# Channel sums of the last stage: two split products over the whole array, or eight unsplit products over two column halves

## The reference

```
def _moe2_ref(x, w_ch1, w_ch2):
    X = np.fft.fft(x, axis=1)
    X = np.fft.fft(X, axis=2)
    u = x + np.real(X)
    mu = np.mean(u, axis=-1, keepdims=True)
    var = np.mean((u - mu) ** 2, axis=-1, keepdims=True)
    un = (u - mu) / np.sqrt(var + 1e-06)
    ch = np.maximum(un @ w_ch1, 0.0) @ w_ch2
    return (u + ch)
```

## Time and profile before

| | |
|---|---|
| median of 3 runs | 1059.18 us (1058.96 to 1059.49) |
| the profiled execution's own time | 1058.91 us |
| its span, first to last instruction | 1057.1 us |
| PE busy | 1032.0 us, 98% of the span, 6896 matmul records |
| PE weight loads busy | 979.6 us, 93% |
| DVE, ACT, POOL busy | 582.2, 502.3 and 413.9 us |
| granted TensorE clock, mean | 0.998 |

### The profile page before, as it was taken

The page is one execution under the profiler, slowest core; times in us unless marked ns, Lnnn a source line. Parts: engine busy times, 40 slices in busy tenths (PEclk is TensorE's granted clock), DMA queues, the critical chain, the costliest instruction groups (busy, mean ns, idle before and its releaser), DMA issues.

```text
span 1057.1 us, 18202 instructions
## 1 busy us (share of the span) xinstructions
PE 1032.0 (98%) x6896; PEld 979.6 (93%) x6896; DVE 582.2 (55%) x1135; ACT 502.3 (48%) x1252; POOL 413.9 (39%) x363
## 2 busy tenths in 40 slices
PE   6899999999999999999999999999999999999998
PEld 5898899999999999999999999888888888888998
DVE  6998995467875477784465687443124114114111
ACT  5989775656875646875656643221111121111110
POOL 5878784343664434573423247331211211111000
PEclk9999999999999999999999999999999999999999
DMA  8636111023302032301123137102001000100000
GB/s 242 198 89 193 44 47 54 6 85 123 104 25 60 1 123 85 104 25 37 36 79 111 45 123 276 41 1 72 1 1 40 33 1 37 35 1 3 34 1 35
DMA packets 41271, 70.08 MB, mean 66 GB/s; under 512 B 6624, under 2 KB 22368, under 8 KB 40672
## 3 DMA queue, kind: packets, MB, share of 16 engines
q1 hardware_dynamic: 40880, 68.59, 20.5%
q10 hardware_dynamic: 304, 0.33, 0.1%
HBM read 56.50 MB, written 12.41 MB: 65 GB/s over the span
## 4 chain that ended last, share of the span: by engine, by line
PE 84%; DVE 6%; POOL 3%; issue 3%; ACT 3%; DMA 0%; DVEq 0%; SPq 0%; ACTq 0%; POOLq 0%
PE PB L840 21%; PE PB L841 21%; PE PB L842 21%; PE PB L905 8%; PE PB L867 6%; PE PB L885 5%; DVE probs L1442 3%; PE PB L907 1%; DVE neg_s L1427 1%; ACT probsT L1169 1%; PE PB L990 1%; ACT exps L1160 0%; POOL k_lo L696 0%; POOL q_hl L689 0%; DMA k_raw<-kT_dram 0%
## 5 line engine op out<-in xcount | busy, mean ns | idle before, releaser
L1386 ACT ACTIVATE h_hi<-PB 128x464 fp32r<-128x464 f32 (+1 forms) x80 | 44.4, 555 | 329.9 <-PE PB L842 329.9
L1665 DVE SCALAR_TENSOR_TENSOR h_lo<-PB,h_hi 128x464 fp32r<-128x464 f32 (+1 forms) x80 | 51.0, 638 | 256.7 <-ACT h_hi L1386 256.7
L1442 DVE SCALAR_TENSOR_TENSOR probs<-neg_s,thresh,exps 128x576 f32<-128x576 f32 x144 | 159.5, 1107 | 0.5 <-ACT exps L1160 0.2
L905 PE MATMUL PB<-v_sb,probsT 128*128 128x64 f32 (+1 forms) x1152 | 146.1, 270 | 0.0
L905 PEld LDWEIGHTS PB<-v_sb,probsT 128*128 128x128 f32 x1152 | 140.8, 193 | 0.0
L1427 DVE TENSOR_SCALAR_CACHE_REDUCE neg_s<-PB,taus 128x576 f32<-128x576 f32 x144 | 117.0, 812 | 40.0 <-PE PB L867 35.6
L1169 ACT ACTIVATE probsT<-PB 128x256 f32<-128x256 f32 (+1 forms) x288 | 103.7, 417 | 71.4 <-PE PB L885 70.7
L842 PE MATMUL PB<-un_h,w1l 128*128 128x464 f32 (+1 forms) x320 | 118.8, 371 | 0.0
L841 PE MATMUL PB<-h_lo,w2h 128*128 128x464 f32 (+1 forms) x320 | 118.8, 371 | 0.0
L840 PE MATMUL PB<-h_hi,w2h 128*128 128x464 f32 (+1 forms) x320 | 118.8, 371 | 0.0
L842 PE MATMUL PB<-h_hi,w2l 128*128 128x464 f32 (+1 forms) x320 | 118.8, 371 | 0.0
(11 more groups left out here) (204 smaller groups left out, 2429.3 us busy)
## 6 DMA issues: line engine op xcount, KB each, us to landing
q_raw<-qT_dram SPq DMA_DIRECT2D x62, 160.0 KB, 3.1
k_raw<-kT_dram SPq DMA_DIRECT2D x64, 144.0 KB, 3.2
w_raw<-w_dram SPq DMA_DIRECT2D x8, 1024.0 KB, 8.4
u_scr<-x2T SPq DMA_DIRECT2D x4, 1152.0 KB, 4.8
cd<-cd_scr SPq DMA_DIRECT2D x4, 1032.0 KB, 5.1
v_sb<-v_dram SPq DMA_DIRECT2D x16, 256.0 KB, 3.1
u_in<-u_scr SPq DMA_DIRECT2D x4, 928.0 KB, 5.1
out_dram<-u_in SPq DMA_DIRECT2D x16, 232.0 KB, 2.1
```

The lines of the kernel that those rows point to most:

```text
L905: last = nc.tensor.matmul(both[:, own], probsT[:, n % 2, kt * P128:(kt + 1) * P128], v_sb[:, kt, pair % 2, own], start=jj in (0, TAIL) and ...
L1442: nc.vector.scalar_tensor_tensor(probs[:, n % 2, place_of(n):place_of(n) + S], neg_s[:, n % 2, :], thresh[:, col:col + 1], exps[:, n % 2, ...
L1665: nc.vector.scalar_tensor_tensor(h_lo[:, ft % 3, 0:w], bank(4 + ft % 3)[:, 0:w], 0.0, h_hi[:, ft % 3, 0:w].bitcast(F32), ALU.max, ALU.subt ...
```

## The change

For chunks 1 to 4 POOL no longer rounds and splits the sum; `add_tiles` ends with the third addition. `over_channels` takes the unsplit float32 `part[:, 0]` and the unsplit `mean512`, and makes eight products in place of two: the columns in four quarters (116, or 112 in the last chunk), and in each quarter first the upper 64 columns of the weights into PSUM partitions 0 to 63, then the lower 64 into partitions 64 to 127. Every product is a group of its own (start and stop). The semaphores count two steps for a chunk after the first. Chunk 0 keeps its two products.

```
 def add_tiles(src, done, c):
...
-                    pool.wait_ge(done, c * 4 + 1)
+                    pool.wait_ge(done, c * 2 + 3)
                     nc.gpsimd.tensor_tensor(part[:, 0, 0:w], part[:, 0, 0:w], part[:, 1, 0:w], ALU.add).then_inc(done, 1)
-                    pool.wait_ge(done, c * 4 + 2)
-                    rounded(part_h[:, 0:w], part[:, 0, 0:w]).then_inc(done, 1)
-                    pool.wait_ge(done, c * 4 + 3)
-                    nc.gpsimd.tensor_tensor(part_l[:, 0:w], part[:, 0, 0:w], part_h[:, 0:w].bitcast(F32), ALU.subtract).then_inc(done, 1)
...
                 def over_channels(c):
                     w = width_of(c)
-                    nc.tensor.matmul(mean_out(c), mean512[:, :].bitcast(F32R), part_h[:, 0:w], start=True, stop=False)
-                    return nc.tensor.matmul(mean_out(c), mean512[:, :].bitcast(F32R), part_l[:, 0:w], start=False, stop=True)
+                    if c == 0:
+                        nc.tensor.matmul(mean_out(c), mean512[:, :].bitcast(F32R), part_h[:, 0:w], start=True, stop=False)
+                        return nc.tensor.matmul(mean_out(c), mean512[:, :].bitcast(F32R), part_l[:, 0:w], start=False, stop=True)
+
+                    for quarter in range(4):
+                        cols = slice(quarter * w // 4, (quarter + 1) * w // 4)
+                        for half in range(2):
+                            rows = slice(half * DH, (half + 1) * DH)
+                            last = nc.tensor.matmul(mean_out(c)[rows, cols], mean512[:, rows], part[:, 0, cols], start=True, stop=True)
+                    return last
...
-                    pe.wait_ge(sums, c * 4 + 4)
+                    pe.wait_ge(sums, c * 2 + 4)
...
-                    pe.wait_ge(sq_sums, c * 4 + 4)
+                    pe.wait_ge(sq_sums, c * 2 + 4)
```

## The result

The changed kernel takes 1065.68 us, median of 3 runs (1064.67 to 1066.59), against 1059.18: ratio 1.0053, 95% interval 1.004 to 1.0067. It is slower, by 6.5 us where 5.0 were forecast. One execution of the kernel before, of 1770.72 us at a mean clock of 0.671, stands beside e9 to e12 and is left out of their ratios.

What follows compares the result with a forecast made beforehand. PE's summed work was taken to bound chunks 0 to 4; per call 0.91 + 0.07 + 0.07 - 0.42 = 0.63 us more, eight calls 5.0 us, forecast 1064.2 us (0.48% slower), range 1062.2 to 1070.2.

Steps and rivals of the forecast that it cites:

- What bounds the kernel: Chunk 0 to chunk 4: PE's summed work sets the end, busy 350.00 of 350.00 us; other engines have time to spare.
- POOL's loss is worth nothing: POOL's sums, ready 1.9 us earlier per call, were already 4.8 us early for PE's product; costed at nothing.
- What PE loses: Two 464-column products per call on PE fall away, giving back 0.42 us.
- The stream of one record: Each unsplit 116-column record on PE streams in 0.101 us, a column costing about two fp32r columns.
- The weight load: Loads of 64 weight columns on PE: 0.053 us each, one after another 0.84 us for 16; profiled duration about 136 ns.
- Side by side: The two halves' records overlap on PE: 0.91 us a call including one record's lead; chance 0.56.
- The changes of kind: Going into and out of each call's unsplit half products on PE: 0.07 us each way.
- The rule of the Trainium skill: Tiling-mode change drains the TensorE, estimated 0.053 us, twice a call: 0.9 us over eight calls, forecast 1064.0 by it alone.
- One after another: Rival: the calls' half records don't overlap on PE, 1.34 us a call, 10.7 us, 1069.9 us; chance 0.30.
- Worse: Rival: weight loads on half arrays aren't hidden, 2.18 us a call, 17.5 us, 1076.7 us; chance 0.06.
- No change: Rival: loads and streams run in pairs, records stream once, 0.42 us a call as taken away, 1059.2 us; chance 0.05.
- Faster: Rival: POOL's chain through mean and `center` is on the path, 1.9 us back per sum, 1049 us; chance 0.02.

Runs made afterwards that it cites:

- e9: Kernel before, plus two unsplit 16-column products on column halves behind each of the eight calls' pairs: 1063.47 us, ratio 1.003.
- e12: Against e5: PE multiplies the rounded sum once on the whole array instead of twice, low part left out for chunks 1 to 4: 1058.11 us, ratio 0.9983.
- e4: Changed kernel with one unsplit 464-column product on the whole array per call in place of eight on halves: 1062.76 us, ratio 1.0026.
- e7: Changed kernel with the eight products of each call issued twice in a row, same result: 1071.65 us, ratio 1.0116.
- e5: Kernel before with POOL's rounding and rest removed; PE still makes two whole-array fp32r products, both with the rounded sum: 1059.48 us, ratio 1.0003.
- e6: Changed kernel with columns cut into eighths (58 columns) instead of quarters, 16 products and 32 records a call: 1066.64 us, ratio 1.0066.
- e2: Changed kernel with the same eight products reordered, four quarters of the upper half first, then four of the lower: 1069.12 us, ratio 1.0088.
- e3: Changed kernel without the four lower-half products of each call: 1065.33 us, ratio 1.0051.
- e8: Changed kernel with two uncut 464-column products per call, upper half then lower half, in place of quarters: 1065.04 us, ratio 1.0054.
- e11: Kernel before with its two split fp32r products going into the upper 64 partitions only, weights of 64 columns: 1059.3 us, ratio 0.999.
- e10: Kernel before, plus one unsplit 16-column product on the whole array behind each of the eight calls' pairs: 1062.25 us, ratio 1.0018.

## Why the prediction was right, point by point

- **What bounds the kernel.** Right: PE 350.00 of 350.00 us before and after, and what e4, e7, e9 and e12 added to or took from PE came out in the h stretch.
- **POOL's loss is worth nothing.** Right, shown by e5: 1.0003 (0.9995 to 1.0011).
- **What PE loses, 0.42 us a call.** Right: taking one of the two products away gives 0.2 us a call (e12).
- **The stream of one record, 0.101 us.** Right within a few per cent: 0.098 (e7: 0.78 / 8, and the step of the pairs).
- **The weight load.** Its duration was put at 136 ns and is 137 (median of L916). That loads of both halves would go one after another, 0.84 us in all, was not so: they run in pairs, and 32 of them fit into 0.93 us (e6). The sum didn't use this term, but it was taken as a floor, and the 0.78 measured lies below it.
- **Side by side.** Right, shown by e2, e3 and the pairs in the count. Its size was put at 0.91 us with one record's lead, where it is 0.78: both halves start at once (the counts of the changed kernel and of e8).
- **The changes of kind, 0.14 us.** This is the term that was mis-sized. It measured 0.35 to 0.38: 0.10 on the way in, 0.05 within the first pair and 0.20 to 0.23 on the way out, all independent of the work between (e9). PEld's rows give the parts: a pause of about 0.1 us on each side, and a load that isn't hidden, of 64 columns going in (0.05) and of 128 going out (0.105). The prediction had no pause and counted the way in as one load that can't be hidden, at 0.07. It took the way back behind unsplit products on the whole array as the price, and let the 33-column products bear on the way in. The first was the wrong kind, and e4 has next to nothing of it; the second are fp32r products, and e11 shows that such products have no edge with 64 columns either.
- **The rule of the Trainium skill** (TensorEngine Tiling (Array Packing), Key Properties) that a change of tiling mode drains the TensorE was the better guide than my reading of rows 9. By e9 and e10 the trace agrees with it: an edge exists for halves and not for the whole array. The estimate of 0.053 us for each drain, worked out from the Trainium skill's page TensorE: Matmul & The Clock Gate, was too low: the pause alone is about 0.1 us on each side, and with the loads that it leaves uncovered the two sides take 0.35 us or more. The same section of the Trainium skill also says that tiles load and multiply in parallel; e3, e6 and e8 agree. The Trainium skill, page PSUM — Partial Sum Buffer, section The four PSUM rules, remarks that float32r products force the full column mask, which fits e11 and the even steps of rows 9.
- **The sum.** 0.78 + 0.37 - 0.42 = 0.73 us a call where 0.63 was forecast: 0.13 too much inside and 0.23 too little at the edges, with opposite signs. That the forecast came so near is in part luck; with the inside as it was put and the edges as they are, it would have been 0.86 us a call and 1066.1 us, still in the range. 5.8 us of the 6.5 are the calls; 0.7 are the early clock, which stood in no term. The prediction called itself wrong if the eight gaps don't add up to the difference of the times. Within the stage they do, and between executions with the same mean clock they do within 0.2 us; between the two medians they don't.
- **The rivals.** One after another, 10.7 us, is refuted by e3. Worse fails too, as the loads run in pairs under the streams (its sum, 8 x 2.18, is 17.4 us and not 17.5). No change fails on the interval and on e4, where a record streams its columns at two cycles each. Faster fails on e5.

## What to carry to other kernels

Splitting an unsplit product over two halves of the array buys nothing when the whole array was full anyway: the halves run at once, but each does half of the work at the same pace, and going over and back cost 0.35 to 0.38 us each time, whatever was done there. Where the accuracy allows one product on rounded data, that is the cheapest (0.21 us against 0.42 for the split pair, 0.8 for the unsplit product and 1.15 on halves). When PE is busy in every microsecond of a stage, hidden work taken from another engine is worth nothing, and a product added to PE costs its full step. These prices are those of this stage, at the high level of the clock.

## What was not expected of the hardware

- Records of two halves start together even where the program's order has the second record of one half between them (e8: two records under way from the first moment), and in e2 the lower half's first record starts beside the upper half's fifth.
- The edges around unsplit products on halves: 0.10 us in, 0.05 in the first pair, 0.20 to 0.23 out, with 16 columns (e9) as with 464. The first load on the halves and the first one behind them don't start under the product in front, as all others around them do.
- An fp32r product with 64 weight columns and 64 output partitions costs what one with 128 costs, 0.20 to 0.21 us at 448 columns, and pays no edge (e11).
- The clock between 109 and 117 us, behind the same 2.0 us wait, is at 1.2 GHz for a longer or shorter time from one execution to the next (granted 0.82 in the profile of before, 0.58 in that of the changed kernel), worth 1.3 us of the whole kernel between the two kinds of execution.
